# RWKV attention, soft MoE and FFN in one fp32 kernel on one core: the slot matrix M made in two column pieces and spread in four, the experts' first layers taken two experts at a time

## The reference

```python
slot_input = (d.T @ x).reshape(E, S_per_e, D)
for e in range(E):
    h = np.maximum(slot_input[e] @ w1[e], 0.0)
    slot_out[e] = h @ w2[e]
x = c @ slot_out                       # c: softmax over the 32 slots
h = x @ w_in
g = h * (1.0 / (1.0 + np.exp(-1.702 * h)))
out = g @ w_out
```

## Time and profile before

| | |
|---|---|
| median of 3 executions | 404.63 us (403.53 to 405.27) |
| the profiled execution | 403.24 us, of which the span from first to last instruction is 401.4 us |
| TensorE (PE) busy in the span | 387.7 us, 97% |
| VectorE, ScalarE, GpSimd busy | 58%, 47%, 28% |
| experts, M, start of the FFN | 142.8 to about 188 us of the span |

### The profile page before, as it was taken

How to read it: one execution, slowest core, us unless ns; L and a number is a source line. 1 busy time by engine, 2 the same in 40 slices (tenths; PEclk the granted TensorE clock), 3 DMA queues, 4 the chain that set the end, 5 groups by cost and what they waited for, 6 DMA issues and landing times.

```text
span 401.4 us, 9106 instructions
## 1 busy us (share of the span) xinstructions
PE 387.7 (97%) x3234; PEld 308.1 (77%) x3234; DVE 234.8 (58%) x423; ACT 188.1 (47%) x432; POOL 111.7 (28%) x113
## 2 busy tenths in 40 slices
PE   4879999999999999999999999999999999999996
PEld 4768888888887744577888888888888888888885
DVE  7667777777778220148565655556565555656551
ACT  1053444444443413376656445554654555456452
POOL 5678777777755021015330000000000000000000
PEclk9599999999999999999999999999999999999999
DMA  7799999999999969980002000200010020002002
GB/s 236 281 376 397 347 327 308 324 321 320 324 301 356 373 214 379 410 293 2 1 0 78 2 0 2 78 0 0 15 63 0 0 78 0 0 0 78 2 0 78
DMA packets 28613, 63.89 MB, mean 159 GB/s; under 512 B 2640, under 2 KB 16576, under 8 KB 28208
## 3 DMA queue, kind: packets, MB, share of 16 engines
q1 hardware_dynamic: 27600, 63.12, 44.2%
q10 hardware_dynamic: 992, 0.49, 0.6%
HBM read 58.88 MB, written 4.72 MB: 158 GB/s over the span
## 4 chain that ended last, share of the span: by engine, by line
PE 89%; DMA 4%; DVE 2%; SPq 1%; issue 1%; POOL 1%; ACT 1%; DVEq 0%; POOLq 0%
PE bank L569 16%; PE bank L571 16%; PE bank L570 16%; PE bank L329 5%; PE bank L360 5%; PE bank L354 5%; PE bank L556 5%; PE bank L347 3%; PE bank L381 3%; PE bank L495 3%; PE bank L476 3%; DMA krb<-kr 2%; DMA rkb<-rk 2%; PE bank L372 2%; PE bank L390 2%; PE bank L404 1%
## 5 line engine op out<-in xcount | busy, mean ns | idle before, releaser
L794 DVE TENSOR_TENSOR gf<-bank,sg 128x512 f32<-128x512 f32 x96 | 66.3, 692 | 86.2 <-ACT sg L945 85.8
L569 PE MATMUL bank<-glo,whi 128*128 128x512 f32 x288 | 112.4, 390 | 0.2 <-DVE glo L800 0.2
L571 PE MATMUL bank<-ghi,wlo 128*128 128x512 f32 x288 | 112.1, 389 | 0.0
L570 PE MATMUL bank<-ghi,whi 128*128 128x512 f32 x288 | 112.0, 389 | 0.0
L945 ACT ACTIVATE sg<-bank 128x512 f32<-128x512 f32 x96 | 57.3, 598 | 93.9 <-PE bank L556 93.9
L800 DVE TENSOR_TENSOR glo<-gf,ghi 128x512 fp32r<-128x512 f32 x96 | 69.4, 723 | 0.2
L569 PEld LDWEIGHTS bank<-glo,whi 128*128 128x128 f32 x288 | 54.1, 188 | 12.3 <-DVE glo L800 1.2
L571 PEld LDWEIGHTS bank<-ghi,wlo 128*128 128x128 f32 x288 | 54.1, 188 | 11.3
L570 PEld LDWEIGHTS bank<-ghi,whi 128*128 128x128 f32 x288 | 54.1, 188 | 11.1
L951 ACT ACTIVATE ghi<-gf 128x512 fp32r<-128x512 f32 x96 | 59.9, 624 | 0.9 <-DVE gf L794 0.9
L837 ACT ACTIVATE yt<-bank 112x512 f32<-112x512 f32 x24 | 14.3, 598 | 65.0 <-PE bank L360 65.0
(11 more groups left out here) (121 smaller groups left out, 390.1 us busy)
## 6 DMA issues: line engine op xcount, KB each, us to landing
ring<-w SPq DMA_DIRECT2D x24, 512.0 KB, 5.8
rkb<-rk SPq DMA_DIRECT2D x23, 512.0 KB, 5.0
krb<-kr SPq DMA_DIRECT2D x24, 384.0 KB, 5.2
ring<-w SPq DMA_DIRECT2D x4, 1536.0 KB, 13.9
ring<-w SPq DMA_DIRECT2D x8, 768.0 KB, 10.7
vb<-v SPq DMA_DIRECT2D x24, 192.0 KB, 5.1
out<-ob SPq DMA_DIRECT2D x18, 256.0 KB, 2.1
ring<-win SPq DMA_DIRECT2D x3, 1024.0 KB, 14.1
```

Source lines behind the costliest of these rows:

```text
L569: pe.matmul(o, w_hi, lo, start=(f == 0), stop=False)
L570: pe.matmul(o, w_hi, hi, start=False, stop=False)
L571: pe.matmul(o, w_lo, hi, start=False, stop=(f == KF - 1)).then_inc(prod_ps, 1)
L794: dve.tensor_tensor(gf[:, f % 2, :], bank[f % 4][:, :], sg[:, f % 2, :], ALU.mult).then_inc(gf_ok, 1)
```

## The change

**Experts.** A bank now holds both column halves of two experts, so the first `h_ps` says that experts 0 and 1 are done. The second layers find their rows at another place in `ht`. The loads of w2, w_in and w_out wait for `h_ps` 1 to 4 one after the other.

**M.** Of each row group's 512 columns the first 128 (`FIRST`, in `LG`) are made first, by 12 matmuls of 128 columns. The other 384 (`REST`, in `YN`) are made in three sets of four matmuls (k = 0, 1, 2) that stand apart. M is spread in four pieces of 8 matmuls of 128 columns: piece 0 before the FFN, pieces 1, 2 and 3 inside tile 0 at f = 1, 4 and 8. The FFN's blocks are numbered so that blocks 4a to 4a+3 are piece a's columns of the four row groups; w_out's rows are loaded in that order. The keep_warm runs have 2 and 10 matmuls instead of 7 and 10. ScalarE copies pieces 1 to 3 in front of the sigmoids of f = 4, 7 and 11.

```diff
+            sp.wait_ge(h_ps, 1)
+            load_half(EG + 1, 0)
+            load_half(EG + 2, 0)
             sp.wait_ge(h_ps, 2)
-            for half in range(2):
-                for e in range(EG + 1, E):
-                    load_half(e, half)
-            sp.wait_ge(h_ps, 4)
+            load_half(EG + 3, 0)
+            for e in range(EG + 1, E):
+                load_half(e, 1)
+            sp.wait_ge(h_ps, 3)
             for k in range(KD):
                 sp.dma_start(win_sb[:, k, :], win[k * P:(k + 1) * P, :]).then_inc(win_in[k], 16)
...
+            for i in range(E // 2):
+                for k in range(KD):
+                    for j in range(4):
+                        e, half = 2 * i + j // 2, j % 2
+                        last = pe.matmul(bank[i][32 * j:32 * j + 32, :], snt[:, k, :],
+                                         ring[:, e, k * FE + 512 * half:k * FE + 512 * half + 512],
+                                         start=(k == 0), stop=(k == KD - 1))
+                last.then_inc(h_ps, 1)
...
+            def m_rows(to, cols, k):
                 pe.wait_ge(win_in[k], 16)
                 for q in range(4):
...
+                if k == KD - 1:
+                    last.then_inc(m_ps, 1)
+            def spread_m(a):
+                for q in range(4):
+                    to = (bank[3], bank[5])[q // 2] if a == 0 else LG
+                    o = slice(128 * (q % 2), 128 * (q % 2) + 128) if a == 0 else slice(128 * q, 128 * q + 128)
+                    t = slice(128 * a, 128 * a + 128)
+                    pe.matmul(to[:, o], spr[:, 0, q, :], mhl[:, 0, t], start=True, stop=False)
+                    last = pe.matmul(to[:, o], spr[:, 1, q, :], mhl[:, 1, t], start=False, stop=True)
+                    if q % 2 if a == 0 else q == 3:
+                        last.then_inc(mst_ps, 1)
+            for k in range(KD):
+                m_rows(LG, FIRST, k)
+            m_rows(YN, REST, 0)
             pe.wait_ge(ct_ok, B + 2)
-            keep_warm(bank[3], 7)
+            keep_warm(bank[0], 2)
             pe.wait_ge(mhi_ok, 1)
             pe.wait_ge(mlo_ok, 1)
-            for q in range(4):
-                pe.matmul(bank[MB[q]][:, :], spr[:, 0, q, :], mhl[:, 0, :], start=True, stop=False)
-                pe.matmul(bank[MB[q]][:, :], spr[:, 1, q, :], mhl[:, 1, :], start=False, stop=True)\
-                  .then_inc(mst_ps, 1)
+            spread_m(0)
+            m_rows(YN, REST, 1)
...
             for f in range(LEAD):
                 hidden(0, f)
-            keep_warm(LG, 10)
+            m_rows(YN, REST, 2)
+            keep_warm(bank[4], 10)
...
+                    if f == 1:
+                        pe.wait_ge(mhi_ok, 2)
+                        pe.wait_ge(mlo_ok, 2)
+                        spread_m(1)
+                        product(0, f)
+                        hidden(0, f + LEAD)
+                        continue
+                    if f in (4, 8):
+                        pe.wait_ge(mst_ok, f // 4 + 1)
+                        spread_m(f // 4 + 1)
...
+                    if not before and f in (4, 7, 11):
+                        a = (f + 1) // 4 if f > 4 else 1
+                        act.wait_ge(mst_ps, a + 2)
+                        act.activation(mst[:, 4 * a * P:(4 * a + 4) * P], LG[:, :], ACT.Copy).then_inc(mst_ok, 1)
```

More of the change, by code:

```diff
@@ L36 @@
 PK = KF // PARTS
+FIRST = slice(0, P)
+REST = slice(P, 4 * P)
 QK = KF // 4
@@ L494, in outputs_of @@
                             pe.wait_ge(w2_in[e], 16)
-                        last = pe.matmul([YN, LG][g][32 * j:32 * j + 32, 0:DM], ht[:, g, k, 32 * j:32 * j + 32],
+                        rows = 32 * (2 * (j % 2) + half)
+                        last = pe.matmul([YN, LG][g][32 * j:32 * j + 32, 0:DM],
+                                         ht[:, g, 4 * (j // 2) + k % 4, rows:rows + 32],
                                          ring[:, W2_AT[e], k * DM:(k + 1) * DM], start=(k == 0), stop=(k == KE - 1))
@@ L571, in product, with first_tile @@
                     pe.matmul(o, w_lo, hi, start=False, stop=(f == KF - 1)).then_inc(prod_ps, 1)
-            pe.wait_ge(mst_even, 1)
             for f in range(LEAD):
                 hidden(0, f)
-            keep_warm(LG, 10)
-            pe.wait_ge(mst_even, 2)
-            pe.wait_ge(mst_odd, 2)
+            m_rows(YN, REST, 2)
+            keep_warm(bank[4], 10)
+            def first_tile():
+                for f in range(KF):
+                    if f % PK == 0:
+                        pe.wait_ge(wlo_ok, f // PK + 1)
+                    if f == 1:
+                        pe.wait_ge(mhi_ok, 2)
+                        pe.wait_ge(mlo_ok, 2)
+                        spread_m(1)
[3 more added lines that the diff above has]
+                    if f in (4, 8):
+                        pe.wait_ge(mst_ok, f // 4 + 1)
+                        spread_m(f // 4 + 1)
+                    if f + LEAD < KF:
+                        hidden(0, f + LEAD)
+                    else:
+                        hidden(1, f + LEAD - KF)
+                    product(0, f)
             def tile(i, more):
                 for f in range(KF):
-                    first = isinstance(i, int) and i == 0
-                    if first and f % PK == 0:
-                        pe.wait_ge(wlo_ok, f // PK + 1)
                     if f + LEAD < KF:
@@ L781, in _, with m_low @@
             dve.tensor_copy(sot[:, :, :].rearrange("p m s -> p (m s)"), YN[:, 0:KD * SLOTS]).then_inc(sot_ok, 1)
[L782 to L786, removed]
+            def m_low(piece):
+                dve.wait_ge(mhi_ok, piece + 1)
+                to, cols = ((LG, FIRST), (YN, REST))[piece]
+                dve.tensor_tensor(mhl[:, 1, cols], to[:, 0:cols.stop - cols.start], mhl[:, 0, cols], ALU.subtract)\
+                   .then_inc(mlo_ok, 1)
+            m_low(0)
+            dve.wait_ge(mst_ps, 2)
+            dve.tensor_copy(mst[:, 2 * P:4 * P], bank[5][:, 0:2 * P]).then_inc(mst_half, 1)
             def product(i, f):
@@ L933, in _, with m_high @@
             act.activation(rsum, rsum, ACT.Sigmoid).then_inc(sig_in, 1)
-            act.wait_ge(m_ps, 1)
-            act.activation(mhl[:, 0, :], LG[:, :], ACT.Copy).then_inc(mhi_ok, 1)
+            def m_high(piece):
+                act.wait_ge(m_ps, piece + 1)
+                to, cols = ((LG, FIRST), (YN, REST))[piece]
+                act.activation(mhl[:, 0, cols], to[:, 0:cols.stop - cols.start], ACT.Copy).then_inc(mhi_ok, 1)
+            m_high(0)
             high_wout(0)
-            for q in (0, 2):
-                act.wait_ge(mst_ps, q + 1)
-                act.activation(mst[:, 512 * q:512 * q + 512], bank[MB[q]][:, :], ACT.Copy).then_inc(mst_even, 1)
+            act.wait_ge(mst_ps, 1)
+            act.activation(mst[:, 0:2 * P], bank[3][:, 0:2 * P], ACT.Copy).then_inc(mst_ok, 1)
             def sigmoid(i, f):
@@ L962, in tile @@
                         high(i, f - 1)
+                        if not before and f == 1:
+                            m_high(1)
                     elif before:
```

29 lines of the change are left out of this document (17 added, 12 removed).

## The result

The changed kernel's median is 406.4 us (405.32 to 407.57, 15 runs), that of the kernel before, timed beside it, 405.02 us (403.53 to 405.92, 15 runs). The ratio is 1.0043, with a 95% interval of 1.003 to 1.0057; it is estimated from all the runs, and the quotient of the two medians, 1.0034, lies in the interval. The changed kernel is slower by 0.4%. Forecast were 406.1 us, slower by 0.37%. The profiled execution took 405.34 us, its span is 403.5 us.

A forecast was written before the change was run, and what follows sets the result against it. TensorE was taken as the bound, running almost without a pause from the experts on. Product 3 coming 0.30 us earlier and 1.84 us for two later pieces gave +1.5 us on 404.63, so 406.1 us, range 403.9 to 409.3.

The forecast's parts named there:

- The experts, 0 us: Experts two at a time: same 10.51 us, loads up to one group sooner; 0 us, 0.3 us at most.
- The first rounding: ScalarE's rounding of M's first piece follows table load and small sigmoid; spread starts at 173.99 instead of 175.35.
- A narrow spread matmul, 0.115 us: Spread of M: 32 matmuls of 128 columns at 0.115 us take 3.7 us, where eight wide ones took 1.92.
- The rival at an fp32 matmul's price: Spread of M: each narrow matmul takes 0.214 us, 3.2 us on top, +4.7, 409.3 us; chance 0.17.
- the one that goes by columns: Spread of M: narrow matmuls cost 0.06 to 0.08 us, change +0.4 to -0.3 us, about 404.7; chance 0.12.
- Two more visits to 32-column weights, 0.48 us: M on TensorE: two REST sets stand apart, adding two visits of 0.09 + 0.15 us, 0.48 us.
- the filler: TensorE's keep_warm before tile 0: ten kept, 2.14 us, ending at 179.71 in the sum.
- The sum up to product 0: TensorE's queue from the first spread at 173.99 puts product 0 at 180.07, 0.39 us earlier than before.
- Tile 0: Pieces 1 to 3 add 0.92 us each; the first replaces losses, product 3 0.30 us earlier, others cost 1.84 us.
- The rival that the waits stay: Tile 0: the 0.83 us of losses return or a block waits for its copy; +2.3, 406.9 us; chance 0.08.
- The clock: TensorE idle 1.1 us with fewer keep_warm: clock falls to 1.2 GHz, 3 us gives 408 or more; chance 0.03.
- The sum: Whole change: -0.30 + 1.84 = +1.5 us on 404.63 gives 406.1 us, slower by 0.37%.

The follow-up runs named there:

- both halves: Changed kernel without the experts' part: ratio to the kernel before 1.007; kernel before with the experts' part alone: 1.0018.
- table_early: Changed kernel with the sigmoid that loads ScalarE's table moved up behind the last exponentials of the combination weights; ratio to the kernel before 1.0038.
- before_table_early: Kernel before the change, with ScalarE's table load moved up behind the last exponentials of the combination weights; ratio to the kernel before 1.0.
- wide_rest: Changed kernel with REST spread by two 384-column matmuls each at f = 1, 3, 6 and 9; ratio to the kernel before 1.0022.
- m_together: Changed kernel with all of M made before the first spread, without the keep_warm of 2; ratio to the kernel before 1.0034.
- warm_5: Changed kernel with the keep_warm run of 10 in front of tile 0 cut to 5; ratio to the kernel before 1.0021.
- combined: Changed kernel with early table load, two REST sets made after three hidden, keep_warm only 3, REST spread in 384 columns; ratio to the kernel before 0.9967.

## Why the prediction was right, point by point

**The experts, 0 us.** Right by both halves. The first piece of w_out was to land before 173.5 and landed at 171.3 (issued at 153.57, 17.7 us to landing). The reason was incomplete, and "TensorE itself doesn't wait for these loads" holds only with the earlier loads: without them M's first piece waits 0.55 us for w_in, which I had not checked, since I had only looked at w_out. It is hidden by the table load.

**The first rounding.** Right. The spread was to start at 173.99 - 142.78 = 31.21 and did at 31.10. TensorE was to be idle for 1.1 us; its row shows 0.71 us from the modelled end of the last keep_warm, and with 0.214 us for each of the two (172.25 to 172.68) it is 0.99 us. `table_early` shows the cause, and `before_table_early` that it wasn't one before.

**A narrow spread matmul, 0.115 us.** Measured 0.1125, by the doubled spread and by the rows. The rival at an fp32 matmul's price (0.214) and the one that goes by columns (0.06 to 0.08) are both out. With the latter goes, for this case of 4-byte weights, the figure of about 81 ns that the Trainium skill (TensorE: Matmul & The Clock Gate, section "Back-to-back issue gap") gives for a matmul of 128 columns in a sustained stream with weight loads. `wide_rest` shows the other side: at 384 columns the same weights cost 0.17.

**Two more visits to 32-column weights, 0.48 us, and the filler.** The sum up to product 0 came out at 37.29, measured 37.15. In the changed kernel a visit with its set takes from 174.58 (the end of the last narrow matmul's 0.11 us) to the first `hidden` at 175.46, 0.88 us as booked. `m_together` takes both out of the way to product 0 and wins 1.63 us of the booked 1.76, 1.28 of them the sets' own matmuls, which fit into TensorE's idle time; its first `hidden` (177.46) waits for ScalarE's copy of `mst`, which ends at 177.40. `warm_5` shows that the queue, not the chain behind the first `hidden`, placed product 0.

**Tile 0.** Product 3 was to stand at 45.02 and stood at 44.91. The first piece was covered by the waits that it replaced, but for 0.12 us (7.76 us from product 0 to product 3, 7.64 before); behind product 3 the changed kernel takes 1.90 us more than before (211.57 and 209.67 us to the last matmul), where 1.84 had been booked for the other two. `glo` 1 and 2 again took 1.35 and 1.99 us (VectorE, changed kernel):

```profile
178.02 0.69 DVE L848 TENSOR_TENSOR glo<-gf,ghi 128x512 fp32r<-128x512 f32 x1
180.22 1.35 DVE L848 TENSOR_TENSOR glo<-gf,ghi 128x512 fp32r<-128x512 f32 x1
182.32 1.99 DVE L848 TENSOR_TENSOR glo<-gf,ghi 128x512 fp32r<-128x512 f32 x1
```

They ended at 178.71, 181.57 and 184.31, and products 0, 1 and 2 started at 179.72, 182.61 and 185.21, so no product waited. The rival that the waits stay is out for this kernel; it came true in part wherever product 0 was brought nearer to the first `hidden` (`warm_5`, `m_together`, `combined`).

**The clock.** The rival is out: the granted clock of 172.5 to 174.5, with the idle time in it, was 1.00 in the changed kernel. That TensorE stood still for about 1 us there did not lower it.

**The sum.** +1.5 us was forecast and 1.49 measured between the two markers: -0.41 + 1.90 where -0.30 + 1.84 had been booked, so that the agreement to a hundredth is in part two small errors that cancel. What I hadn't seen is +0.8 us at the end, with a fetch of ScalarE's code beside the last stores. No step of mine looked behind the last matmul. The total of +1.74 us (0.43% of 405) is smaller than the 2.3 us that both make, and the interval (1.2 to 2.3 us) takes in 1.5 and just reaches 2.3; the timed runs alone couldn't have told them apart. That 406.1 lies so near to the measured 406.4 is partly luck: the forecast started from 404.63 us, while the kernel before, timed beside, had 405.02, and it left out the end.

## What to carry to other kernels

Cut a chain of matmuls finer only after pricing the piece: a matmul with 128-column 4-byte weights took 0.11 us at 128 columns and 0.17 at 384, so three narrow ones cost twice what a wide one does. Before a first piece is made short to start its followers sooner, look at what else its follower's engine does at that moment; here a table load swallowed 0.95 of the 2.4 us by which the first spread could start sooner, until it was moved. And measure an edit of one stage between two markers in the trace, and the time outside of them apart, or the scatter of another stage and an accident at the end will be taken for the edit.

## What the runs showed of the hardware that was not expected

- A fetch of 8 KB of instructions for ScalarE stood among the last stores of the changed kernel, and those 256 KB stores landed after 2.8 us instead of 2.0. The changed kernel has three counted instructions more on ScalarE. Another 40 moved the fetch from 400 to 234 us and the stores were back at 2.1 us, and 5 in the kernel before moved it from behind the span's end to just before the first store's packets, where it cost nothing.
- Inside tile 0 the first two of eight narrow matmuls start 0.05 us apart (181.77 and 181.82), the others 0.11 to 0.12.
- With the same code in front of them, the experts began between 142.57 and 145.24 us in fourteen traces, more than the whole effect under study.
